# A decayed linear-attention recurrence on TensorE: which operand is stationary, and where the last weights are split

## Chip, core and metric

The kernel runs on one core of a Trainium2 chip. The metric is the time of one execution in device microseconds. Times of stretches are taken from one profiled execution and counted from the start of its span.

## What is computed

Three layers in a row, all in fp32. First a recurrence per batch and head (4 x 8 heads, 768 positions, head dimension 48):

```python
f = 1.0 / (1.0 + np.exp(-f_logit))
for t in range(S):
    state = f[:, :, t, :, None] * state + np.einsum('bhd,bhe->bhde', k[:, :, t], v[:, :, t])
    y[:, :, t] = np.einsum('bhd,bhde->bhe', q[:, :, t], state)
```

Its 3072 rows x of 384 numbers go to a mixture of 8 experts, of which each row takes one:

```python
logits = (x / (norm(x) + 1e-06)) @ (expert_emb / (norm(expert_emb) + 1e-06)).T / tau
expert_idx = np.argmax(logits, axis=1)       # gate_w: its softmax probability
out[mask] = gate_w[mask, None] * (np.maximum(x[mask] @ w1[e], 0.0) @ w2[e])
```

and the result to a bilinear layer: `((x @ w1) * (x @ w2) @ w3) @ w_out`.

## The kernel before, in words

Five engines run programs of their own and meet at semaphores. The recurrence is cut into `NT` = 24 tiles of 128 positions, four batches in turn (`B` = 4), so the state that tile i needs comes from tile i - 4. All 8 heads of a tile are done together, in `NP` = 4 pairs j of two heads g; the two heads of a pair lie in partitions 0 to 47 and 64 to 111. `steps` runs a software pipeline: in step s, TensorE works on scores and products of tile s, cumulative logs of tile s + 2, turning of q and k of tile s + 1 and the output rows of tile s - 1. Each engine has its own `step` with its own order; that order is the queue of the engine.

TensorE's step before, in order: `scores` (stationary kT, 64 rows by 128 columns, moving qT; into two PSUM banks, one for each half of a pair), `cumulate` (running sums of the logs by a triangular matrix), `rows_and_logits` of tile s - 1, `turn_qk` (8 transposes), `state_products`, `update_products` (k times v into `b_s`), `chunk_products`. The output y of a tile is built transposed in the bank `b_y`: the state products have the decayed state (`apart`, 48 columns, the heads of a pair kept apart by zeros) stationary and 128 columns of qT moving; the chunk products have v (48 columns) stationary and the masked scores `am` moving. ScalarE copies this to `yT` (`copy_yT`). `rows_and_logits` makes rows and expert logits of it in one go: yT is stationary, and `pick`, which holds an identity and the expert embeddings, moves with 104 columns. VectorE's `take_rows` copies the rows to `x_ring` and sums the logits; SP stores the rows.

Other names that the steps touch. VectorE: `mask` (scores times the triangle), `bound`, `low_logs`, `copy_kT`, `carry` (new state sum, s_sum), `scale_k` (ks), and `low_w3`. ScalarE: `logs`, `exps`, `copy_qT`, `square` (norms of rows), `high_wo`, `high_w3`. GpSimd: `clamp`, `scale_q` (qs), `decay` (e_half, state and apart from the last row of the decays, which goes by DMA through `last_rows` to `e_all`). SP issues all loads in the order of `stage`; `load_v` waits for the decay of an earlier tile.

Matrices are split in two parts (`_hi`, rounded, and `_lo`, the rest), and `three` multiplies them in three fp32r products. The product w3 @ w_out, `w34_product`, 8 blocks f1 of 24 products, is computed while the routing runs: blocks stand between the steps of the routing in TensorE's order. Its inputs w3 and w_out are loaded and split inside the recurrence's loop: in each step ScalarE makes a half row block high, VectorE the low part. After the recurrence come a flag (whether a decay was too strong, then a slow path), norms (a square root on ScalarE, with a table load), softmax, rank matmuls (L810, L811), lists of rows (L816, L823), gathers by GpSimd, and then the expert slots and the bilinear layer, which the change does not touch.

Of the kernel before, what the change touches and what calls it, by code (L numbers as in the profile page):

```python
# [18 lines left out]
F32 = mybir.dt.float32  # L19
# [17 lines left out]
E = 8  # L37
# [14 lines left out]
TURN_AT = 3  # L52
LISTS = 5
# [11 lines left out]
NORM_AT = 3  # L65
# [9 lines left out]
def steps(eng, step):  # L75

    for s in range(-3, 5):
        step(s, s % 4)
    with eng.Fori(1, NT // 4 - 1) as m:
        for u in range(4):  # L80
            step(m * 4 + (1 + u), (1 + u) % 4, (m, u))
    for s in range(NT - 3, NT + 1):
        step(s, s % 4)
# [24 lines left out]
def build(nc, ctx, qkvf, emb, tau, sets1, sets2, w3_t, w_out, out):  # L108
# [22 lines left out]
    w3_lo = low_w3.enter_context(nc.sbuf_tensor("w3_lo", [P, KF, KF, P], F32R))  # L131
# [7 lines left out]
    def early(name, shape, dt=F32):  # L139
# [3 lines left out]
    early("rest_of_w3_lo", [P, KF * FF - KF * 2 * DM])  # L143
    x_all = early("x_all", [P, (RING + 1) * DM])
    wo_lo = early("wo_lo", [P, KF, DM], F32R)
    above = ExitStack()
    w3_hi = above.enter_context(nc.sbuf_tensor("w3_hi", [P, KF, FF], F32R))
    above.close()
    early("first_w3_hi", [P, FF])
    w3_sb = early("w3_sb", [P, KF, FF])  # L150
# [3 lines left out]
    early("first_wo_hi", [P, DM])  # L154
    wo_sb = early("wo_sb", [P, KF, DM])
    early("up_to_rows", [P, 1216])
# [18 lines left out]
    yT = early("yT", [P, NP * P])  # L175
    state = early("state", [P, B, NP, D])
    apart = early("apart", [P, B, NP, 2, D])
    half = early("half", [P, 2])
    e_half = early("e_half", [P, NP, 2])
# [3 lines left out]
    pick = early("pick", [P, NP, 2 * D + E])  # L183
# [6 lines left out]
    en_sq = early("en_sq", [P, NP, E])  # L190
# [22 lines left out]
    scratch = apart[:].rearrange("p b j g d -> p (b j g d)")  # L213
# [13 lines left out]
    SL = [pick[0:1].rearrange("p j n -> p (j n)")[:, k * (SLOTS + 2) * E:(k + 1) * (SLOTS + 2) * E].rearrange(  # L227
        "p (t e) -> p t e", e=E) for k in range(2)]
# [23 lines left out]
    def mid(name, shape, dt=F32):  # L252
# [17 lines left out]
    bank = [ctx.enter_context(nc.psum_tensor(f"bank{n}", [P, 512], F32)) for n in range(6)]  # L270
    b_cum, b_qT, b_kT, b_y, b_s, b_x = bank
# [16 lines left out]
    w3_hi_done, w3_lo_done = sem("w3_hi_done"), sem("w3_lo_done")  # L288
    masks_done, pads_done = sem("masks_done"), sem("pads_done")
    const_one, const_done, pick_done, emb_turned, en_sq_done, ones_done = (sem(n) for n in (  # L290
        "const_one", "const_done", "pick_done", "emb_turned", "en_sq_done", "ones_done"))
# [5 lines left out]
    sp_done, kv_done, sum_done, half_done, s_done, y_done, yT_done, xl_at = (sem(n) for n in (  # L297
        "sp_done", "kv_done", "sum_done", "half_done", "s_done", "y_done", "yT_done", "xl_at"))
# [1246 lines left out]
```

## Time and profile before

| | |
|---|---|
| median of 3 runs | 728.2 us (727.57 to 729.82) |
| profiled execution | 729.75 us, span 728.0 |
| TensorE busy | 714.8 us, 98% |
| VectorE, ScalarE, GpSimd busy | 350.7, 290.2, 200.3 us |
| granted TensorE clock, mean | 0.997 of full speed |

The page gives the busy time of each engine (PE TensorE, PEld its weight loads, DVE VectorE, ACT ScalarE, POOL GpSimd, SP SyncE), the chain of waits that ended last, and groups of instructions by line. L722 is line 722 of the kernel. The ends of matmuls are modelled, and the durations of neighbours overlap; for a stream of them, the distance from start to start is the cost. The rows below the change are such lines.

### The profile page before, as it was taken

Reading aid. Unit: us, or ns where it says so; the run is one execution under the profiler, and the core shown is the slowest. Engines: PE = TensorE matmul, PEld = TensorE weight load, DVE = VectorE, ACT = ScalarE, POOL = GpSimd, SP = SyncE. Lnnn points to the kernel's source line nnn. Section 1 sums busy time; section 2 is a strip of 40 time slices with the busy share of each in tenths; the row PEclk is TensorE's granted clock in tenths of the full one; section 3 lists DMA queues with packets and bytes.
Section 4 is the critical chain, followed back from the end, with each engine's and each line's share of the span. In section 5 each row is a group of like instructions: output and inputs, shape, how many; then the busy total and the mean of one; then the engine's idle time right before and its main releaser. Section 6 shows DMA issues by size and latency. Waiting matters only on the chain.

```text
span 728.0 us, 14063 instructions
## 1 busy us (share of the span) xinstructions
PE 714.8 (98%) x4911; PEld 655.6 (90%) x4911; DVE 350.7 (48%) x580; ACT 290.2 (40%) x557; POOL 200.3 (28%) x234
## 2 busy tenths in 40 slices
PE   7999999999989999999999999999999999999997
PEld 6999899989989999999999988988988989889887
DVE  6889998768745545455465541211312113112121
ACT  5677788534235534345354442212123022031130
POOL 5756677502320120200000003114033042141242
PEclk9999999999999999999999999999999999999999
DMA  7687886234463454423342440000000000010001
GB/s 220 194 240 212 252 255 158 78 118 122 133 206 96 136 166 131 130 86 109 113 124 86 130 130 1 1 11 33 1 22 22 0 32 11 0 43 0 20 23 43
DMA packets 73057, 70.80 MB, mean 97 GB/s; under 512 B 20520, under 2 KB 61480, under 8 KB 73024
## 3 DMA queue, kind: packets, MB, share of 16 engines
q1 hardware_dynamic: 69952, 60.95, 28.3%
q0 software_dynamic: 3072, 9.44, 4.2%
q8 instruction: 18, 0.29, 0.2%
q14 instruction: 15, 0.12, 0.1%
HBM read 60.88 MB, written 9.49 MB: 97 GB/s over the span
## 4 chain that ended last, share of the span: by engine, by line
PE 82%; DMA 5%; issue 5%; POOL 4%; DVE 2%; SPq 1%; ACT 0%; POOLq 0%; ACTq 0%; DVEq 0%
PE bank L743 14%; PE bank L744 14%; PE bank L745 14%; PE b_a L743 9%; PE b_a L744 9%; PE b_a L745 9%; DMA e_all<-last_rows 4%; PE b_a L673 2%; PE bank L682 2%; PE bank L722 1%; PE bank L702 1%; PE bank L713 1%; POOL apart L554 1%; POOL xs L606 1%; PE bank L834 1%
## 5 line engine op out<-in xcount | busy, mean ns | idle before, releaser
L632 POOL TENSOR_TENSOR p_lo<-prod,p_hi 128x512 fp32r<-128x512 f32 x42 | 53.9, 1283 | 333.3 <-ACT p_hi L1116 333.3
L1113 ACT COPY a_sb<-b_a 128x512 f32<-128x512 f32 x48 | 28.2, 587 | 218.2 <-PE bank L745 218.2
L1494 DVE TENSOR_TENSOR prod<-bank,a_sb 128x512 f32<-128x512 f32 x48 | 33.2, 691 | 165.7 <-ACT a_sb L1113 165.7
L1450 DVE SCALAR_TENSOR_TENSOR h_lo<-b_a,h_hi 128x432 fp32r<-128x432 f32 x64 | 38.8, 607 | 97.2 <-ACT h_hi L1066 97.2
L1066 ACT ACTIVATE h_hi<-b_a 128x432 fp32r<-128x432 f32 x64 | 34.0, 532 | 124.3 <-PE b_a L745 124.0
L1141 DVE TENSOR_TENSOR w_lo<-w_raw,w_hi 128x768 fp32r<-128x768 f32 x72 | 67.9, 956 | 5.3 <-ACT w_hi L1032 1.2
L743 PE MATMUL bank<-h_hi,w_hi 128*128 128x432 f32 x192 | 69.9, 364 | 0.2
L745 PE MATMUL b_a<-x_hi,w_lo 128*128 128x432 f32 x192 | 68.7, 358 | 0.0
L744 PE MATMUL b_a<-x_lo,w_hi 128*128 128x432 f32 x192 | 68.7, 358 | 0.0
L744 PE MATMUL bank<-h_lo,w_hi 128*128 128x432 f32 x192 | 68.7, 358 | 0.0
L745 PE MATMUL bank<-h_hi,w_lo 128*128 128x432 f32 x192 | 68.7, 358 | 0.0
L743 PE MATMUL b_a<-x_hi,w_hi 128*128 128x432 f32 x192 | 68.7, 358 | 0.0
L745 PE MATMUL bank<-w,p_lo 128*128 128x384 f32 x192 | 64.2, 334 | 0.0
L743 PE MATMUL bank<-w,p_hi 128*128 128x384 f32 x192 | 64.2, 334 | 0.0
L744 PE MATMUL bank<-w,p_hi 128*128 128x384 f32 x192 | 64.2, 334 | 0.0
L1032 ACT CAST w_hi<-w_raw 128x768 fp32r<-128x768 f32 x72 | 58.5, 833 | 0.0
L606 POOL DMA_INDIRECT xs<-x_recurrence,ids x24 | 25.9, 1081 | 113.1 <-PE bank L834 80.2
L743 PE MATMUL b_a<-m_hi,w_hi 128*128 128x512 f32 x144 | 56.1, 390 | 0.6 <-DVE w_lo L1141 0.6
L745 PE MATMUL b_a<-m_hi,w_lo 128*128 128x512 f32 x144 | 56.1, 390 | 0.0
L744 PE MATMUL b_a<-m_lo,w_hi 128*128 128x512 f32 x144 | 56.1, 390 | 0.0
L745 PE MATMUL bank<-m_hi,w_lo 128*128 128x512 f32 x144 | 56.0, 389 | 0.0
L744 PE MATMUL bank<-m_lo,w_hi 128*128 128x512 f32 x144 | 56.0, 389 | 0.0
(226 smaller groups left out, 1540.3 us busy)
## 6 DMA issues: line engine op xcount, KB each, us to landing
w_raw<-sets SPq DMA_DIRECT2D x80, 192.0 KB, 3.5
w_raw<-sets SPq DMA_DIRECT2D x40, 384.0 KB, 4.2
ring_all<-qkvf SPq DMA_DIRECT2D x24, 384.0 KB, 4.1
ring_fc<-qkvf SPq DMA_DIRECT2D x24, 192.0 KB, 3.9
ring_all<-qkvf SPq DMA_DIRECT2D x24, 192.0 KB, 3.2
x_recurrence<-x_all SPq DMA_DIRECT2D x24, 192.0 KB, 3.5
w_sb<-w_t SPq DMA_DIRECT2D x8, 512.0 KB, 4.9
wo_sb<-w_out SPq DMA_DIRECT2D x8, 192.0 KB, 4.2
```

Source lines behind the costliest of these rows:

```text
L606: pool.indirect_dma_start(out=xs[:, w % BATCH, :], out_offset=None, in_=rec_dram.rearrange("b c p n -> (b c p) n"), in_offset=bass.Indirec ...
L632: pool.tensor_tensor(p_lo[:, f, :], prod[:, f % 2, :], p_hi[:, f, :].bitcast(F32), ALU.subtract).then_inc(pl_done, 1)
L673: mm = pe.matmul([b_a0, b_a1][g][:, j * P:(j + 1) * P], kT[g * HP:(g + 1) * HP, r % 2, j, :], qT[g * HP:(g + 1) * HP, r % 2, j, :], start= ...
L743: pe.matmul(acc, a_hi, b_hi, start=first, stop=False, skip_group_check=skip)
L744: pe.matmul(acc, a_hi, b_lo, start=False, stop=False, skip_group_check=skip)
L745: return pe.matmul(acc, a_lo, b_hi, start=False, stop=last, skip_group_check=skip)
L1032: act.copy(piece(w_hi, f), piece(w_raw, f)).then_inc(wh_done, 1)
L1066: act.activation(h_hi[:, f % 2, 0:SW], b_h[f % 2][:, 0:SW], ACT.Relu).then_inc(hh_done, 1)
L1113: act.copy(a_sb[:, f % 2, :], b_a[f % 2][:]).then_inc(as_done, 1)
L1141: return dve.tensor_tensor(out_, whole, high.bitcast(F32), ALU.subtract)
L1450: dve.scalar_tensor_tensor(out=h_lo[:, f % 2, 0:SW], in0=b_h[f % 2][:, 0:SW], scalar=0.0, in1=h_hi[:, f % 2, 0:SW].bitcast(F32), op0=ALU.m ...
L1494: dve.tensor_tensor(prod[:, f % 2, :], b_b[f % 2][:], a_sb[:, f % 2, :], ALU.mult).then_inc(pr_done, 1)
```

## The change

- The state products take qT as stationary operand (64 rows by 128 columns) with 48 columns of the undoubled `state` moving; the chunk products take `am` as stationary (128 by 128) with 48 columns of v moving. y comes out in rows, in two banks `b_y0` and `b_y1`. `apart`, `half`, `e_half`, `pick` and `yT` are gone.
- VectorE's `take_rows` copies these rows to `x_ring` straight from the banks. Then `turn_x` transposes them (3 transposes into `b_x`, which `cumulate` uses too), ScalarE copies (`copy_xT_tile`), and a step later `logits` (3 matmuls with the turned rows stationary and 8 columns of embeddings moving) goes into free columns of `b_s`.
- TensorE's order in a step: scores, state products, cumulate, turning of q and k, logits of tile s - 2, turn of the rows of tile s - 1, chunk products, update products. The update of the last four tiles, whose state nobody needs, is left out.
- `scale_k` moves from VectorE to GpSimd (the first tile's stays), which loses two of the three operations of `decay`. `load_v` waits for the update instead of the decay; `load_qk` of a tile is issued one stage later.
- The split of w3 and w_out leaves the loop. w_out is split in two halves in steps 21 to 23 by ScalarE and VectorE (`high_wo`, `low_wo`); w3 in 8 blocks of 1024 columns, high parts by ScalarE from step 21 on and during the routing, low parts by GpSimd, two in the last steps and six ahead of its gathers. Each `w34_product` waits for its own block.
- The flag is found in the last steps, and an extra step NT + 1 holds the last logits.

The core of the diff:

```diff
         def state_products(i, r):
-            need(pe, yT_done, i)
+            need(pe, x_done, i)
             need(pe, s_done, i - B + 1)
             for j in range(NP):
                 for g in range(2):
-                    mm = pe.matmul(b_y[g * HP:g * HP + D, j * P:(j + 1) * P], apart[:, r % 4, j, g, :],
-                                   qT[:, r % 2, j, :], start=(j == 0), stop=False, skip_group_check=True)
+                    mm = pe.matmul([b_y0, b_y1][g][:, j * D:(j + 1) * D], qT[g * HP:(g + 1) * HP, r % 2, j, :],
+                                   state[g * HP:(g + 1) * HP, r % 4, j, :], start=(j == 0), stop=False,
+                                   skip_group_check=True)
             mm.then_inc(sp_done, 1)
...
         def chunk_products(i, r):
             pe.wait_ge(am_done, i + 1)
+            pe.wait_ge(v_landed[r % 4], (i - r % 4) * 4 + 16)
             for j in range(NP):
                 for g in range(2):
                     h = 2 * j + g
-                    mm = pe.matmul(b_y[g * HP:g * HP + D, j * P:(j + 1) * P], ring_v[:, r % 4, h * D:(h + 1) * D],
-                                   am[:, g, j, :], start=False, stop=True, skip_group_check=True)
+                    mm = pe.matmul([b_y0, b_y1][g][:, j * D:(j + 1) * D], am[:, g, j, :],
+                                   ring_v[:, r % 4, h * D:(h + 1) * D], start=False, stop=True, skip_group_check=True)
             mm.then_inc(y_done, 1)
...
-        def rows_and_logits(i):
-
-            pe.wait_ge(yT_done, i + 1)
+        def turned_x(rows):
+            for k in range(KD):
+                mm = pe.transpose(b_x[:, k * P:(k + 1) * P], rows[:, k * P:(k + 1) * P], ident[:])
+            return mm
+
+        def turn_x(i, r):
+
+            pe.wait_ge(x_done, i + 1)
+            pe.wait_ge(bound_done, min(i + 4, NT) if isinstance(i, int) else i + 4)
+            turned_x(x_ring[:, r % 4, :]).then_inc(x_turned, 1)
+
+        def logits_of(acc, xT_rows):
+            for k in range(KD):
+                mm = pe.matmul(acc, xT_rows[:, k * P:(k + 1) * P], en_t[:, k, :], start=(k == 0), stop=(k == KD - 1),
+                               skip_group_check=True)
+            return mm
+
+        def logits(i, r):
+
+            pe.wait_ge(x_copied, i + 1)
+            need(pe, sum_done, min(i + 2, NT - B) if isinstance(i, int) else i + 2)
             need(pe, rl_done, i)
...
+            mm = logits_of(b_s[:, L_AT:L_AT + E], xT_tile[:, r % 2, :])
...
         def step(s, r, part=None):
...
                 scores(i, r)
+                if isinstance(i, int) and i == 0:
+                    pe.wait_ge(pads_done, 2)
+                state_products(i, r)
             if (i := tile_of(s, 2)) is not None:
                 cumulate(i, r + 2)
...
                 turn_qk(i, r + 1)
+            if isinstance(s, int) and s == NT + 1:
+                w34_product(0, range(2, 4))
+            if (i := tile_of(s, -2)) is not None:
+                if isinstance(i, int) and i == 0:
+                    pe.wait_ge(emb_in, 16 * KD)
+                logits(i, r + 2)
+            if isinstance(s, int) and s == NT:
+                w34_product(0, range(2))
+            if (i := tile_of(s, -1)) is not None:
+                turn_x(i, r + 3)
+            if isinstance(s, int) and s == NT:
+                pe.wait_ge(least_done, 1)
+                pe.transpose(b_qT[0:1, 0:P], least_e[:], ident[:]).then_inc(least_turned, 1)
             if (i := tile_of(s, 0)) is not None:
-                if isinstance(i, int) and i == 0:
-                    pe.wait_ge(blank_done, 1)
-                    pe.wait_ge(pads_done, 2)
-                state_products(i, r)
-                update_products(i, r)
                 chunk_products(i, r)
+                if not (isinstance(i, int) and i >= NT - B):
+                    update_products(i, r)
...
+        def scale_k(i, r):
+            if isinstance(i, int) and i == 0:
+                pool.sem_inc(ks_done, 1)
+                return
+            pool.wait_ge(exp_done, i + 1)
+            need(pool, kv_done, min(i - 1, NT - B + 1) if isinstance(i, int) else i - 1)
+            need(pool, tr_done, i - 1)
+            pool.tensor_tensor(ks[:, r % 2, :, 0:D], ring_qk[:, r % 4, DM:2 * DM].rearrange("p (h d) -> p h d", h=H),
+                               en[:, r % 2, :].rearrange("p (h d) -> p h d", h=H), ALU.mult).then_inc(ks_done, 1)
...
+        def low_w3(f1):
+            pool.wait_ge(w3_hi_done, f1 + 1)
+            if f1 >= LOW_HEAD:
+                pool.wait_ge(w3_lo_done, f1)
+            pool.tensor_tensor(w3_lo(f1), w3_raw(f1), w3_hi(f1).bitcast(F32), ALU.subtract).then_inc(w3_lo_done, 1)
...
             if (i := tile_of(s, -1)) is not None:
                 act.wait_ge(x_done, i + 1)
                 need(act, nsq_done, i)
                 square(i, x_ring[:, (r + RING - 1) % RING, :]).then_inc(nsq_done, 1)
-            if part:
-                high_w3(*part)
+            if (i := tile_of(s, 1, 1)) is not None:
+                copy_qT(i, r + 1)
+            if (i := tile_of(s, 2)) is not None:
+                exps(i, r + 2)
+            if (i := tile_of(s, -1)) is not None:
+                copy_xT_tile(i, r + 3)
+            if isinstance(s, int) and s == NT - 3:
+                high_wo(0)
+                high_w3(0)
+            if isinstance(s, int) and s == NT - 2:
+                high_w3(1)
+            if isinstance(s, int) and s == NT - 1:
+                high_wo(1)
+                high_w3(2)
+            if isinstance(s, int) and s == NT:
+                high_w3(3)
```

## Rows read from the trace of the kernel before

**Rows 1.** The page's busy time of TensorE: us, share of the span, instructions.
```profile
PE 714.8 (98%) x4911; PEld 655.6 (90%) x4911; DVE 350.7 (48%) x580; ACT 290.2 (40%) x557; POOL 200.3 (28%) x234
```

**Rows 2.** Busy time by stretches (columns in the first line): first to last scores.
```profile
core 0: us, PE busy (x) PEld busy (x) DVE busy (x) ACT busy (x) POOL busy (x), PEclk, DMA share, GB/s
13.29:144.38 131.09, 130.60 (x1878) 119.60 (x1878) 117.02 (x213) 96.53 (x230) 86.74 (x121) 1.00 0.69 199
```

**Rows 3.** The chain that ended last, one steady step: start us, us, what.
```profile
104.76 1.09 PE b_a L673 x16
105.86 0.38 PE bank L664
106.40 0.87 PE bank L722 x8
107.27 0.87 PE bank L713 x8
108.15 1.01 PE bank L682 x16
109.16 0.45 PE bank L693 x16
109.61 0.88 PE bank L702 x16
```

**Rows 4.** TensorE in order of time: start us, us, instructions; starts of the scores.
```profile
13.29 1.16 PE L673 MATMUL b_a<-qT,kT 64*128 64x128 f32 x16 [0.88 <-DVE kT L1165]
...
35.29 1.16 PE L673 MATMUL b_a<-qT,kT 64*128 64x128 f32 x16
...
41.21 1.16 PE L673 MATMUL b_a<-qT,kT 64*128 64x128 f32 x16
...
87.53 1.16 PE L673 MATMUL b_a<-qT,kT 64*128 64x128 f32 x16 [0.49 <-DVE kT L1165]
...
144.38 1.16 PE L673 MATMUL b_a<-qT,kT 64*128 64x128 f32 x16
```

**Rows 5.** TensorE in order of time, products of the last weights around the rank matmuls.
```profile
156.45 0.33 PE L743 MATMUL b_a<-wo_hi,w_hi 128*128 128x384 f32 x1
...
158.01 0.33 PE L743 MATMUL b_a<-wo_hi,w_hi 128*128 128x384 f32 x1
...
160.11 0.39 PE L810 MATMUL bank<-apart,before 128*128 128x8 f32 x2 [1.42 <-DVE apart L1320]
160.36 0.37 PE L811 MATMUL bank<-apart,ones 128*128 128x8 f32 x2
160.58 0.45 PE L743 MATMUL bank<-wo_hi,w_hi 128*128 128x384 f32 x1
...
163.38 0.53 PE L743 MATMUL bank<-wo_hi,w_hi 128*128 128x384 f32 x1
```

**Rows 6.** Weight loads in order of time, the first of the state products.
```profile
102.35 0.83 PEld L682 LDWEIGHTS bank<-qT,apart 128*48 128x48 f32 x16 [0.17 <-issue]
```

**Rows 7.** VectorE in order of time, at the start.
```profile
5.01 1.22 DVE L1243 COPY pick<-ident 128x384 f32<-128x384 f32 x1
...
6.20 0.51 DVE L1146 TENSOR_TENSOR lg_lo<-lg,lg_hi 128x384 fp32r<-128x384 f32 x1
```

**Rows 8.** GpSimd in order of time, in the steady loop.
```profile
103.50 1.00 POOL L542 TENSOR_TENSOR qs<-ring_all,ec 128x384 f32<-128x384 f32 x1
105.92 0.20 POOL L550 TENSOR_TENSOR e_half<-e_all,half 128x8 f32<-128x8 f32 x1 [1.42 <-DMA e_all<-last_rows]
...
107.34 1.16 POOL L536 TENSOR_SCALAR ring_fc<-ring_fc 128x384 f32<-128x384 f32 x1
```

**Rows 9.** Groups of instructions by line and shape, 0 to 225: busy us, mean ns.
```profile
L1141 DVE TENSOR_TENSOR w_lo<-w_raw,w_hi 128x768 fp32r<-128x768 f32 x16 | 14.9, 953 | 0.8 <-ACT w_hi L1032 0.3
...
L1032 ACT CAST w_hi<-w_raw 128x768 fp32r<-128x768 f32 x16 | 12.6, 834 | 0.0
```

**Rows 10.** ScalarE in order of time, table load and root of the norms.
```profile
154.06 1.28 ACT L1025 ACT_TABLE_LOAD   x1 [1.63 <-DVE flag L1263]
...
155.35 0.23 ACT L1025 ACTIVATE rt<-nsq 128x32 f32<-128x32 f32 x1
```

More of the change, by code:

```diff
@@ L81, in steps @@
             step(m * 4 + (1 + u), (1 + u) % 4, (m, u))
-    for s in range(NT - 3, NT + 1):
+    for s in range(NT - 3, NT + 2):
         step(s, s % 4)
@@ L174, in build @@
     am = early("am", [P, 2, NP, P])
-    yT = early("yT", [P, NP * P])
+    xT_tile = early("xT_tile", [P, 2, DM])
     state = early("state", [P, B, NP, D])
-    apart = early("apart", [P, B, NP, 2, D])
-    half = early("half", [P, 2])
-    e_half = early("e_half", [P, NP, 2])
+    scratch = early("scratch", [P, 8 * NT * E])
     s_sum = early("s_sum", [P, NP, D])
@@ L226, in build @@
         "p (v i) -> p v i", v=3)
-    SL = [pick[0:1].rearrange("p j n -> p (j n)")[:, k * (SLOTS + 2) * E:(k + 1) * (SLOTS + 2) * E].rearrange(
-        "p (t e) -> p t e", e=E) for k in range(2)]
+    SL = [slot_rows[:, k, :].rearrange("p (t e) -> p t e", e=E) for k in range(2)]
     front.close()
@@ L422, in _ @@
         stage(NT // RING - 1, 0)
-        load_v(NT - 3, 1)
-        load_last(NT - 6, 2)
-        save_last(NT - 5, 3)
-        load_qk(NT - 1, 3)
-        for i in range(NT - 4, NT):
-            if i >= NT - 2:
-                load_v(i, i % RING)
+        for i in range(NT - 3, NT):
+            load_v(i, i % RING)
+            load_last(i - 3, (i - 3) % RING)
+            save_last(i - 2, (i - 2) % RING)
+            if i < NT - 1:
+                load_qk(i + 1, (i + 1) % RING)
+        for i in range(NT - 2, NT):
             load_last(i - 1, (i - 1) % RING)
@@ L441, in _ @@
         with sp.If(trips == 1):
-            for k in range(KD):
-                sp.dma_start(en_t[:, k, :], emb[:, k * P:(k + 1) * P].rearrange("e p -> p e"),
-                             allow_slow_non_contiguous=True).then_inc(emb_turned, 16)
             with sp.Fori(0, CH) as c:
@@ L579, in step @@
                 before_clamp(i, r + 3)
[L580 removed]
+            if (i := tile_of(s, -2)) is not None and not (isinstance(i, int) and i >= NT - B):
                 decay(i, r + 2)
@@ L609, in gather @@
                 ).then_inc(gathered, 16)
+        for f1 in range(2, KF):
+            low_w3(f1)
         pool.wait_ge(x_done, NT)
@@ new lines, in take_logits, with low_wo @@
+        def take_logits(i):
+            return dve.tensor_copy(row_of(i), b_x[:, DM:DM + E])
+        def low_wo(half):
+            rows = slice(half * KF // 2, (half + 1) * KF // 2)
+            dve.wait_ge(wo_hi_done, half + 1)
+            low(wo_lo[:, rows, :], wo_sb[:, rows, :], wo_hi[:, rows, :]).then_inc(wo_lo_done, 1)
+        def step(s, r, part=None):
+            if (i := tile_of(s, -1)) is not None:
+                take_rows(i, (r + RING - 1) % RING)
+                if not (isinstance(i, int) and i >= NT - B):
+                    carry(i, r + 3)
+            if isinstance(s, int) and s == NT:
+                for q in range(RING):
+                    dve.wait_ge(last_landed[q], 16 * (NT // RING))
+                dve.tensor_reduce(least_e[:], e_all[:].rearrange("p i j -> p (i j)"), AXX, ALU.min
+                                  ).then_inc(least_done, 1)
```

273 lines of the change are left out of this document (119 added, 154 removed).

## The prediction

> **What bounds the kernel now.** I read the page's busy line first: TensorE is busy over nearly the whole span [rows 1]. A share of that kind is an average, so next came the busy time by stretches: from the first scores to those of the last tile TensorE idles 0.5 us of 131.09, at the full clock, VectorE 14, ScalarE and GpSimd 35 and more [rows 2]. The third view is the chain in the steady loop. It runs down TensorE alone, part after part, and one step of it (one tile of 128 positions) takes from 104.76 to 109.61 + 0.87 = 110.48, so 5.72 us [rows 3]. The starts of the scores confirm it: 13.29 for the first tile, 144.38 for the last, and one stall of 0.49 at 87.53 because the copy of kT came late [rows 4]. So in the recurrence every us of TensorE work added to a step is a us on the end; work taken from the other engines is worth nothing beyond that one stall. After the recurrence TensorE fills the routing with products of the last weights, with one real idle time, 1.42 us before the rank matmuls [rows 5].
>
> **The rate that decides.** An fp32 matmul stands in the trace as two pairs of load and matmul. The 8 instructions of `rows_and_logits` move 104 columns each and take 0.87 us, 0.109 each; the 8 transposes move 128 columns and take 0.87 to 0.88, also 0.109 [rows 3]. With fewer columns the price hardly falls: the extra matmul with `ones` stationary moves 32 columns in two instructions, and its step takes 41.21 - 35.29 = 5.92 instead of 5.72, so 0.10 each [rows 4]; with 8 columns, L810 and L811 take 0.25 and 0.22 for two each, 0.118 on average (the next products are longer, so the second pair may already have met the slower clock) [rows 5]. What these have in common is a stationary operand of 128 rows by 128 columns in fp32. I read it as the load of that operand setting the pace: 0.109 (0.100 to 0.118) per instruction, whatever moves, up to 128 columns. Where two small tiles share the array the price is lower: scores, 64 rows by 128 stationary, 16 in 1.09; state products, 48 stationary columns with 128 moving, 16 in 1.01; chunk products likewise, 0.88; update, 64 stationary columns with 48 moving, 16 in 0.45, 0.028 each [rows 3].
>
> The Trainium skill (TensorE: Matmul & The Clock Gate, LDWEIGHTS) says that a load's time goes by its columns at 1.2 per ns, 107 ns for 128. The trace agrees for the full array, with 0.109. By that figure the sixteen chunk products would be an estimated 1.71 us. The Trainium skill (TensorEngine Tiling (Array Packing), When to Use Tiling) also advises, for a small free dimension, to make the small operand stationary and tile the columns. The kernel before does just that, at 0.88 us, and the change undoes it; by the page alone the change would lose up to a factor of two on these products.
>
> **The change part by part, in one steady step.**
> - Scores: untouched, 1.09. Of it about 0.18 is the pause after products of another tile shape, as before the state products (0.17 idle, issue) [rows 6].
> - State products: still 16 instructions, but the stationary operand is now qT, 64 rows by 128, with 48 state columns moving. Bounds: 0.45 (update row) and 16 x 0.109 = 1.74 (loads of the two halves one after another). The scores have the very same stationary shape and take 1.09 with 128 moving, so the halves do overlap. They follow the scores in the same shape: 1.09 - 0.18 = 0.91, against 1.01 before.
> - Cumulate 0.54, turning of q and k 0.88: the same.
> - `rows_and_logits` goes, -0.87. In its place `turn_x`, 3 transposes: 3 x 0.109 = 0.33, and `logits`, 3 matmuls, 6 instructions with 8 columns: 6 x 0.109 = 0.65. Bounds of the latter 0.17 (6 x 0.028, update row) and 0.71 (6 x 0.118).
> - Chunk products: am becomes stationary, 128 x 128 over the full array, 48 columns move. Bounds 0.45 and 16 x 0.118 = 1.89; 16 x 0.109 = 1.74 by the nearest rows, those of the full array with few columns. Before, 0.88. This is the main term.
> - Update: now behind a full-array group, so it takes the pause: 0.45 + 0.17 = 0.62.
>
> Sum: 1.09 + 0.91 + 0.54 + 0.88 + 0.33 + 0.65 + 1.74 + 0.62 = 6.76 us against 5.72.
>
> The first step lacks turn and logits, the second the logits: 5.78 and 6.11. Steps 2 to 19: 18 x 6.76 = 121.68, and 0.20 for the matmul of the norms. The last four tiles have no update: steps 20 and 21 are 6.14 each, step 22, without cumulate, 5.60. From the first to the last scores this is 151.65 against 131.09: **+20.56**.
>
> **Start.** VectorE's memset of yT and its 1.22 us copy into pick stand ahead of lg_lo; lg_lo started at 6.20, right behind that copy [rows 7]. The chain of waits goes through lg_lo, so what it gains is between 0 and the 1.2 of the copy, less what ScalarE's lg then holds up; I take -0.4. The three emb DMAs that replace eight shorten SP's queue, which nobody waits for here. **Stall at 87.53:** -0.5, since VectorE loses the weight split and scale_k.
>
> **What moves to other engines, at nothing.** VectorE was busy 117.02 us over these 23 steps [rows 2], 5.1 each, and loses more than it gains, of 6.76. Its order holds: take_rows needs the chunk products and has the update and scores (1.7 us) to finish before the state products ask for it. GpSimd loses e_half and apart and gains scale_k: the whole decay before took 107.34 - 105.92 = 1.42, clamp 1.16, qs 1.00, ks about the same, so at most 4.6 us [rows 8]. It works a step ahead: its decay began 1.2 us behind the scores at 104.76, for a turning that comes in the next step. By the order of the new step that turning wants ks 2.5 us in, 9.3 us behind those scores. GpSimd would be through after 5.8; 3.5 us are free. On SP, load_v waits for the update instead of for the decay, which comes earlier; load_qk moves one tile nearer, but is issued more than a step ahead of its use. If the GpSimd cover is gone, each us is a us of the step.
>
> **The tail.** T is the start of the last scores. Before: rank matmuls at 160.11 - 144.38 = T+15.7. Now TensorE works 4.72 to the end of the chunk products. The second half of the w_out split sits in the queues in front of the last rows: ScalarE copies the turned rows of the tile before by T+3.8, then high_wo(1), 1536 elements, twice the 0.83 of 768: T+5.4; VectorE's low_wo(1) waits for it and takes twice 0.95 [rows 9]: T+7.3. Only then take_rows, T+7.9. TensorE, with the logits and six products (0.173 each, nine in 1.56 [rows 5]) done at T+6.4, waits 1.5. Turn, square and copy until T+9.2, high_w3(3) about 1.1, the flag's read about 1 and a table load 1.28: the root at T+12.6, before at T+11.0 [rows 10]. The chain from there to the rank matmuls is unchanged: **+1.6**. Whether the slow clock after the wait (nine products in 2.80 after 160.58 [rows 5]) comes again is open; about 1.5 us less if not. GpSimd's blocks of w3_lo, 1024 elements, some 2.5 us each, stand in front of its gathers. TensorE takes 24 x 0.173 = 4.2 us per block, so they keep ahead; the last ends near T+26.5, the ids come near T+28.5. Slack 2 us, then a us per us.
>
> Total: 20.56 + 1.6 - 0.4 - 0.5 = **+21.3 us**. The profiled execution took 729.75 around its span of 728.0, so its like would be 751.0; the median of the runs is 728.2, and against it the forecast is **749.5**.
>
> **Rivals.**
> - *The load hides, faster.* If a load for full-array products overlapped as in the update row, 0.028 per instruction, chunk and state would be 0.45 each, logits 0.17: a step of 4.53. VectorE and ScalarE then limit at about 5: 24 x (5.0 - 5.72) = -17, time 711. The rest of the step sums to 4.04, so with 25 full-array instructions it turns into a gain once one costs under (5.72 - 4.04) / 25 = 0.067. Nothing above shows it that cheap in fp32; the rows at 8 and 32 columns speak directly against it. 7 in 100 with its milder forms, up to 727.
> - *The two halves of the state products don't overlap.* 1.74 instead of 0.91: 0.83 x 24 = 20 more, 769 to 770. Against it the scores row. 5 in 100.
> - *ks from GpSimd becomes the wait.* It decides if the last-row DMA lands more than 4.7 us behind the scores; it let the decay go at 1.2. With half a us per step, 12 more: 761. 7 in 100.
> - *The change does what it says and the time doesn't show it:* needs the step within 0.1 of 5.72, chance 1 in 100.
>
> **How the numbers follow.** The forecast has 80 in 100. Its own bounds: at 0.100 per instruction, state products 0.85 and no pause before the update, a step is 6.3: 10 less, 739; at 0.118, with the state products at the scores' 1.09, 7.1: 8 more, 758. The range 738 to 760 holds this case nearly whole, and the milder half of a wait on ks. Faster by over 0.3% (about what a measurement of this kernel can tell from no change) has 0.07, within 0.3% 0.02, slower 0.91.
>
> **What would show it.** Chunk products with 16 instructions in 1.6 to 1.9 us; logits near 0.65; state products near 0.9; scores 6.3 to 7.1 us apart; TensorE still without idle time in the loop; and VectorE and ScalarE idler. A step below 5.7 refutes the rate; idle time of TensorE ahead of the ks transposes, the queue reading; a first-to-last distance of 152 with a time outside the range, the tail.

## The result, and the profile of the changed kernel

The changed kernel takes 769.2 us (median of four runs, 767.65 to 769.85), the kernel before 728.0 beside it. The ratio is 1.0558, with an interval from 1.0534 to 1.0582: slower by 41.2 us, where the forecast was slower by 21.3 and the range ended at 760. The profiled execution took 769.85 around a span of 768.0, against 729.75 around 728.0.

The page's busy line and its row of TensorE's granted clock, which answer to [rows 1]:

```profile
PE 748.4 (97%) x4887; PEld 695.3 (91%) x4887; DVE 332.2 (43%) x519; ACT 286.1 (37%) x535; POOL 212.4 (28%) x212
PEclk9999999977899999999999999999999999999999
```

TensorE is as full as before. The clock row says more: three of the 40 slices, from 154 us on, show 7, 7 and 8 tenths. There the recurrence ends and the routing begins.

The chain that ended last, one steady step (start us, us, what), which answers to [rows 3]:

```profile
105.19 1.09 PE b_a L689 x16
106.28 0.83 PE b_y L698 x16
107.10 0.38 PE bank L680
107.48 0.18 PE bank L681
107.66 0.87 PE bank L733 x8
108.53 0.57 PE bank L750 x6
109.10 0.38 PE bank L739 x3
109.48 1.72 PE b_y L721 x16
111.20 0.60 PE bank L711 x16
111.80 1.09 PE b_a L689 x16
```

A step is 111.80 - 105.19 = 6.61 us, before 5.72. Its parts are scores, state products (L698), cumulate, turning of q and k (L733), logits (L750), turning of x (L739), chunk products (L721), update (L711). TensorE alone carries it, as before.

The changed kernel by stretches (each row: us, busy time and instruction count of TensorE, weight loads, VectorE, ScalarE, GpSimd, then the granted clock, DMA share and GB/s), which answers to [rows 2]:

```profile
14.00:152.00 138.00, 137.81 (x1734) 133.38 (x1732) 84.42 (x146) 78.21 (x188) 79.05 (x94) 1.00 0.63 181
...
158.00:160.00 2.00, 0.74 (x14) 0.55 (x10) 0.00 (x0) 1.12 (x2) 0.87 (x2) 1.00 0.44 116
...
162.00:166.00 4.00, 4.00 (x22) 3.91 (x22) 1.52 (x4) 0.61 (x2) 0.00 (x0) 0.50 0.10 36
...
182.00:184.00 2.00, 2.00 (x15) 2.00 (x14) 0.56 (x3) 1.43 (x2) 0.30 (x1) 0.92 0.00 0
```

In the loop TensorE has no idle time worth naming and the full clock; VectorE and ScalarE are at six tenths of it. Then, at 158, TensorE stands still for a while, and from 162 to 182 its clock is at half (0.50, 1.2 GHz). It falls to half twice more, each time behind a wait: for some 6 us behind the one before the rank matmuls, and for some 3 us from 220 on.

The same from TensorE's rows in order of time (start, us, line, operation, what ended the idle time before it): the scores of the last three tiles, the first work after the standstill, and the rank matmuls. They answer to [rows 4, 5]:

```profile
13.54 1.16 PE L689 MATMUL b_a<-qT,kT 64*128 64x128 f32 x16 [0.88 <-DVE kT L1197]
...
151.56 1.16 PE L689 MATMUL b_a<-qT,kT 64*128 64x128 f32 x16
...
157.58 1.16 PE L689 MATMUL b_a<-qT,kT 64*128 64x128 f32 x16
160.99 1.23 PE L698 MATMUL b_y<-state,qT 64*128 64x48 f32 x16 [2.25 <-DVE x_all L1217]
...
169.15 2.08 PE L689 MATMUL b_a<-qT,kT 64*128 64x128 f32 x16
...
192.86 0.59 PE L838 MATMUL bank<-scratch,before 128*128 128x8 f32 x2 [2.47 <-DVE scratch L1358]
```

The scores of tile 21 in the kernel before, the same view:

```profile
133.29 1.16 PE L673 MATMUL b_a<-qT,kT 64*128 64x128 f32 x16
```

So the surplus over the kernel before grows like this. At the scores of tile 21 it is 151.56 - 133.29 = 18.3. At those of tile 23 it is 169.15 - 144.38 = 24.8 [rows 4]. At the rank matmuls it is 192.86 - 160.11 = 32.8 [rows 5], and at the end 768.0 - 728.0 = 40.0. The loop costs about what the forecast said. The other half of the loss arises in its last two steps and behind them, where the forecast had put 1.6.

Two readings of the trace name candidates. The first is the chain of waits ahead of the standstill (start us, us, what); SPq is SyncE's queue:

```profile
156.46 1.16 DMA last_rows<-ec
...
157.64 0.40 SPq L362
...
158.08 2.23 DMA x_recurrence<-x_all
...
160.38 0.57 DVE x_all L1217
```

VectorE's copy of tile 21's rows (L1217) goes into the ring slot of tile 17 and must wait until that is stored. The store stands in SyncE's queue behind all loads of the loop and behind both DMAs of tile 23's last rows, which themselves wait for an exp. So it starts only at 158.08. TensorE needs the bank that the copy empties.

The second is VectorE beside GpSimd during the routing. VectorE, in order of time:

```profile
190.09 2.71 DVE L1358 TENSOR_TENSOR_SCAN scratch<-restart,scratch 128x192 f32<-128x192 f32 x1
...
193.08 1.91 DVE L1363 TENSOR_SCALAR rt<-rt 128x24 f32<-128x24 f32 x1
195.03 0.30 DVE L1364 RECIPROCAL gates<-rt 128x24 f32<-128x24 f32 x1
...
195.57 1.92 DVE L1368 TENSOR_TENSOR_SCAN rt<-ones,rt 128x8 f32<-128x8 f32 x1
...
197.73 2.27 DVE L1370 TENSOR_TENSOR rt<-rt 128x8 f32<-128x8 f32 x1
```

GpSimd, the same time, with the splits of blocks 4 to 7 of the last weights:

```profile
190.03 4.92 POOL L569 TENSOR_TENSOR w_lo_head<-w_all,w_high 128x1024 fp32r<-128x1024 f32 x2 [3.95 <-ACT w_high L1011]
195.10 4.87 POOL L569 TENSOR_TENSOR w_high<-w_all,w_high 128x1024 fp32r<-128x1024 f32 x2
```

In the trace of the kernel before the same four instructions run with GpSimd idle:

```profile
159.50 0.56 DVE L1320 TENSOR_TENSOR_SCAN apart<-restart,apart 128x192 f32<-128x192 f32 x1
...
160.34 0.18 DVE L1325 TENSOR_SCALAR rt<-rt 128x24 f32<-128x24 f32 x1
...
161.09 0.17 DVE L1330 TENSOR_TENSOR_SCAN rt<-ones,rt 128x8 f32<-128x8 f32 x1
...
161.50 0.17 DVE L1332 TENSOR_TENSOR rt<-rt 128x8 f32<-128x8 f32 x1
```

Here they take 2.71, 1.91, 1.92 and 2.27, together 7.7 more. Each of them ends about when an instruction of GpSimd does (the two of the first row at about 192.5 and 195.0, those of the second at about 197.5 and 200.0). The reduce, the reciprocal and the copy out of PSUM (195.36, 0.17) are not stretched.

The rule stands in the Trainium skill (SBUF — State Buffer, SBUF: two separate sides): VectorE and GpSimd share a pair of ports as "an **exclusive lock**, not a bandwidth split", taken on VectorE's side by an instruction in a two-port mode or, against a GpSimd instruction that reads SBUF, by one with two SBUF inputs, and held for a whole instruction. The trace agrees: the four end with GpSimd's instructions, and the reduce and the reciprocal, with one input, and the copy that reads PSUM keep their durations.

### The profile page after: what moved, and what is told of

Its sections match the earlier page's. It is cut to its first block, busy times and chain, and to the rows that moved or that the text cites. A ratio compares the mean times of both kernels' runs of the same rounds, so it can differ in the third digit from the quotient of the medians.

```text
span 768.0 us, 13790 instructions
## 1 busy us (share of the span) xinstructions
PE 748.4 (97%) x4887; PEld 695.3 (91%) x4887; DVE 332.2 (43%) x519; ACT 286.1 (37%) x535; POOL 212.4 (28%) x212
## 4 chain that ended last, share of the span: by engine, by line
PE 87%; issue 4%; DVE 4%; POOL 1%; DMA 1%; ACT 1%; ACTq 0%; DVEq 0%; POOLq 0%; SPq 0%
PE b_a L768 9%; PE b_a L770 9%; PE b_a L769 9%; PE bank L770 8%; PE bank L768 8%; PE bank L769 8%; PE b_y L721 6%; PE b_y L768 5%; PE b_y L770 5%; PE b_y L769 5%; PE b_a L689 3%; PE bank L733 3%; PE b_y L698 3%; PE bank L750 2%; PE bank L711 2%
## 5 line engine op out<-in xcount | busy, mean ns | idle before, releaser
L1488 DVE SCALAR_TENSOR_TENSOR h_lo<-b_a,h_hi 128x432 fp32r<-128x432 f32 x64 | 38.8, 606 | 97.2 <-ACT h_hi L1106 95.8
L768 PE MATMUL bank<-m_hi,w_hi 128*128 128x512 f32 x144 | 56.0, 389 | 0.0
L721 PE MATMUL b_y<-ring_all,am 128*128 128x48 f32 x384 | 48.4, 282 | 0.0
L721 PEld LDWEIGHTS b_y<-ring_all,am 128*128 128x128 f32 x384 | 48.1, 204 | 0.0
L768 PE MATMUL b_y<-h_hi,w_hi 128*128 128x432 f32 x128 | 46.9, 367 | 0.9 <-DVE h_lo L1488 0.6
L770 PE MATMUL b_y<-h_hi,w_lo 128*128 128x432 f32 x128 | 45.8, 358 | 0.0
L769 PE MATMUL b_y<-h_lo,w_hi 128*128 128x432 f32 x128 | 45.8, 358 | 0.0
```

The lines of the kernel that those rows point to most:

```text
L721: mm = pe.matmul([b_y0, b_y1][g][:, j * D:(j + 1) * D], am[:, g, j, :], ring_v[:, r % 4, h * D:(h + 1) * D], start=False, stop=True, skip_ ...
L768: pe.matmul(acc, a_hi, b_hi, start=first, stop=False, skip_group_check=skip)
L769: pe.matmul(acc, a_hi, b_lo, start=False, stop=False, skip_group_check=skip)
L770: return pe.matmul(acc, a_lo, b_hi, start=False, stop=last, skip_group_check=skip)
L1488: dve.scalar_tensor_tensor(out=h_lo[:, f % 2, 0:SW], in0=b_h[f % 2][:, 0:SW], scalar=0.0, in1=h_hi[:, f % 2, 0:SW].bitcast(F32), op0=ALU.m ...
```

## The experiments

Those named a_ start from the changed kernel, those named b_ from the kernel before. Ratios are against the kernel before, run on the same chip, with their interval.

**The load's rate.** Eight more fp32 matmuls a step, with the 128 x 128 identity stationary and 8, 48 or 128 columns moving; they go into a bank that the state products start afresh.

```
+                need(pe, yT_done, i)
+                for _ in range(8):
+                    pe.matmul(b_y[:, 0:8], ident[:], upto[:, 0:8], start=True, stop=True)
```

> The kernel before with 8 more fp32 matmuls per step, stationary 128 by 128, only 8 columns moving. Theory (the load sets the pace): the same 41.9 us more as with 48 columns, span 770. Rival (by moving columns, with a floor): 3 to 11 us more, span 731 to 739.

> The kernel before with 8 more fp32 matmuls in each of its 24 steps, stationary 128 by 128, 48 columns moving, into a bank that is overwritten afterwards. Theory (the load of a 128 by 128 fp32 operand sets the pace at 0.109 per instruction): 16 x 0.109 x 24 = 41.9 us more, span 770. Rival (cost goes by the columns that move, 128 columns in 0.109): 16 x 0.041 x 24 = 15.7 us more, span 744; at the update row's 0.028, 10.8 more.

> The kernel before with 8 more fp32 matmuls per step, stationary 128 by 128, 128 columns moving. Both theories: 16 x 0.109 x 24 = 41.9 us more, span 770, since 128 moving columns take as long as the load. If load and moving were added instead of overlapped: twice as much, span 812.

One run each: 769.5, 768.2 and 770.2 us. The chain shows the sixteen added instructions (L784) in one steady step, with 8 columns and then with 128:

```profile
105.02 1.69 PE bank L784 x16
```

```profile
105.36 1.79 PE bank L784 x16
```

From the first to the last scores the three kernels take 169.4, 170.2 and 171.7 us, against 131.1 before, so 38.3, 39.1 and 40.6 more. Over 23 steps with 16 instructions that is 0.104, 0.106 and 0.110 for each. Sixteen times as many moving columns add 0.006. So for these shapes the columns that move do not set the pace, as the forecast had it, and its 0.109 was slightly too dear for few columns. What the three share is the stationary operand of 128 by 128, whose load the forecast named. Whether it is the load itself, or another cost of every instruction that fills the array, no run separates.

**The orientation of the chunk products alone.**

```
-                    mm = pe.matmul(b_y[g * HP:g * HP + D, j * P:(j + 1) * P], ring_v[:, r % 4, h * D:(h + 1) * D],
-                                   am[:, g, j, :], start=False, stop=True, skip_group_check=True)
+                    mm = pe.matmul(b_y[:, h * HP:h * HP + D], am[:, g, j, :],
+                                   ring_v[:, r % 4, h * D:(h + 1) * D], start=False, stop=True, skip_group_check=True)
```

> The kernel before with one part of the change: the chunk products alone take the masked scores as stationary operand (128 by 128) and move 48 columns of v; they are written in rows into the same bank, so that y, and all that follows, is not the reference's. Theory (0.104 to 0.110 per full-array instruction): 1.66 to 1.76 instead of 0.88 us per step, and up to 0.17 for one more change of tile shape: 24 x (0.8 to 1.05) = 19 to 25 us more, 748 to 753 us. Rival (half the moving columns is a gain): 728 or less.

Measured: 837.3 us, far off. The steady step in the chain of waits, though, shows what was asked:

```profile
103.88 1.92 PE bank L702 x16
```

Sixteen products with 1.92 instead of 0.88: +1.04 a step, of which the pause after products of another tile shape is about 0.2 (1.72 in the changed kernel, where they follow the same shape). Over 23 steps the first and last scores lie 154.5 apart, 23.4 more. The remaining 86 of the 109 us come from the expert stage: with rows that are not y, the routing fills more slots. The page's group of the hidden layer's split, which has x64 and 38.8 us in the kernel before:

```profile
L1450 DVE SCALAR_TENSOR_TENSOR h_lo<-b_a,h_hi 128x432 fp32r<-128x432 f32 x88 | 53.4, 607 | 129.0 <-ACT h_hi L1066 129.0
```

At eight instructions a slot that is 11 slots instead of 8. The run's time says nothing of the change; its step does. That was a fault of the experiment's plan: its expectation took the time downstream as independent of the data.

**The place of the stores.** Each ring slot's store goes up into the last three steps of SyncE's loop.

```
         for i in range(NT - 3, NT):
 ...
             if i < NT - 1:
                 load_qk(i + 1, (i + 1) % RING)
+            store_x((i - RING) // B, (i - RING) % B)
 ...
-        for i in range(NT - 7, NT):
+        for i in range(NT - 4, NT):
```

> The changed kernel with one move on SP's queue: the stores of the rows of tiles 17, 18 and 19 stand right behind the loads of tiles 21, 22 and 23, instead of behind all loads and the last rows' round trips. Theory (the copy of tile 21's rows waited 4.6 us for a ring slot whose store was queued too late, TensorE idled 2.3 us for it, and its clock then stayed at half until 182): the wait goes, 2.3 us and about 10 us of half clock come back, 757 us, spacing of the last scores about 6. Rival (the wait was for the rows' own chain and another wait takes its place, or the clock falls all the same at the light end of the recurrence): 766 to 769 us.

Measured: 757.2 us, ratio 1.0401 (1.0377 to 1.0425). By the ratios that is 11.4 us less than the changed kernel, by the medians 12.0, as expected. TensorE's rows around the former standstill:

```profile
158.24 0.99 PE L699 MATMUL b_y<-state,qT 64*128 64x48 f32 x16
...
162.85 1.16 PE L690 MATMUL b_a<-qT,kT 64*128 64x128 f32 x16
```

No wait, and the full clock up to the last scores (162.85 instead of 169.15). From 168 the clock falls here too (0.50 until 170, 0.68 until 172, then 1.00). The wait of 2.25 us cost 11 to 12 mainly because the steps behind it ran at half clock: the mean granted clock of the four runs is 0.976 to 0.979 in the changed kernel and 0.991 to 0.995 here, and 0.015 of 760 us is an estimated 11 us.

**GpSimd's lock, three ways.** First, its splits in four instructions of 256 columns instead of one of 1024.

```
-            pool.tensor_tensor(w3_lo(f1), w3_raw(f1), w3_hi(f1).bitcast(F32), ALU.subtract).then_inc(w3_lo_done, 1)
+            for q in range(0, KF, 2):
+                ins = pool.tensor_tensor(w3_lo(f1)[:, q:q + 2, :], w3_raw(f1)[:, q:q + 2, :],
+                                         w3_hi(f1)[:, q:q + 2, :].bitcast(F32), ALU.subtract)
+            ins.then_inc(w3_lo_done, 1)
```

> The changed kernel with GpSimd's split of each block of 1024 columns made as four instructions of 256 columns, same place, same work. Theory (an exclusive lock: a VectorE instruction with all operands in SBUF waits until the GpSimd instruction that has begun is over): the four stretched instructions of the rank chain (2.71, 1.91, 1.92, 2.27 us instead of 0.56, 0.18, 0.17, 0.17) lose most of their 7.7 us of waiting, at most 0.6 each is left; 6 to 8 us faster, 761 to 763. Rival (the two engines share a bandwidth): the GpSimd work is the same, so the chain is stretched as much as before, 769 us.

> Both edits. If the steady loop (scores 6.62 to 6.76 us apart against 5.72) is all that the orientation of the products costs, and the rest of the loss stood in these two places: 769 - 12 - 7 = 750 us, the forecast's number. If something else at the end costs as well: 755 us or more. If the two hide each other: about 757.

Measured: 766.6 (1.0534, 1.0512 to 1.0556) alone, 754.8 (1.0385, 1.0358 to 1.0412) together with the stores' new place, so by the medians 2.6 and 2.4 us less, a third of what was expected, and by the ratios only 1.7 and 1.2, with intervals that overlap. Nor did both edits give the 750 that was expected of them. VectorE in order of time, of the kernel with the pieces alone:

```profile
191.60 1.09 DVE L1361 TENSOR_TENSOR_SCAN scratch<-restart,scratch 128x192 f32<-128x192 f32 x1
...
194.68 0.66 DVE L1372 TENSOR_TENSOR rt<-rt 128x8 f32<-128x8 f32 x1
...
196.08 0.85 DVE L1375 TENSOR_TENSOR scratch<-scratch,rt 128x192 f32<-128x192 f32 x1
```

The single waits are short now, but there are many: the two engines take turns, piece against instruction, and what took 0.17 to 0.36 takes 0.66 to 0.85, ten times over.

Second, the splits of blocks 4 to 7 left out altogether (the products take the high parts in place of the low ones), with the stores in their new place.

```
+            if f1 >= 4:
 ...
+                pool.tensor_tensor(w3_lo(f1)[:, 0, 0:8], w3_raw(f1)[:, 0, 0:8], w3_hi(f1)[:, 0, 0:8].bitcast(F32),
+                                   ALU.subtract).then_inc(w3_lo_done, 1)
+                return
```

> The changed kernel with the stores moved as before, and GpSimd's split of w3 blocks 4 to 7 left out (a token of 8 columns stays for the order; the third product of each of these blocks takes the high part instead of the low one, same shape, so the output lacks their low part). Theory (the pieces only gave way to more collisions, twelve of 0.5 us instead of four of 2; what counts is that GpSimd works in SBUF beside the rank chain at all): all stretched instructions of the chain fall back to 0.17 to 0.56, 7.7 us and one idle time of TensorE with its half clock come back, 748 us (747 to 750). Rival (the rank chain does not set the end, TensorE's products do): 755 us or more.

Measured: 748.0 us, 1.0261 (1.0238 to 1.0284), so 10.2 us less by the ratios than with the stores' place alone, 9.2 by the medians. VectorE's chain has its old durations back:

```profile
180.54 0.56 DVE L1365 TENSOR_TENSOR_SCAN scratch<-restart,scratch 128x192 f32<-128x192 f32 x1
...
181.37 0.18 DVE L1370 TENSOR_SCALAR rt<-rt 128x24 f32<-128x24 f32 x1
```

GpSimd's own queue is no rival for this price: with the stores' place alone, its splits end at 189.1, and its first gather, at 198.78, waits for VectorE's ids.

Third, the same splits made later, after the lists of positions are out.

```
-        for f1 in range(2, KF):
+        for f1 in range(2, 4):
+            low_w3(f1)
+        pool.wait_ge(list_in, 1)
+        for f1 in range(4, KF):
             low_w3(f1)
```

> The changed kernel with the stores moved, and GpSimd's blocks 4 to 7 held back until VectorE has made the list of the rank chain, nothing left out. Theory: the chain is free, but the fifth product waits about 1.8 us for its block, the gathers start some 7 us later and VectorE's later instructions collide instead: between the two, 750 to 754 us. Rival: the held blocks and late gathers cost more than the chain gains, 757 us or more.

Measured: 756.6, 1.0381 (1.0359 to 1.0404): almost nothing against 1.0401, and above the 750 to 754 that was expected. The chain up to the rank matmuls is free of the lock. The held splits then meet VectorE's later instructions, of which one (L1407) takes 2.76 us, and the gathers of GpSimd stand behind them. Of this kernel, VectorE's row with the ids, and then a row of GpSimd's splits and its first gather:

```profile
192.74 0.60 DVE L1404 CAST ids<-rt 128x4 int32<-128x4 f32 x1
```

```profile
193.46 5.29 POOL L570 TENSOR_TENSOR w_high<-w_all,w_high 128x1024 fp32r<-128x1024 f32 x2
198.92 1.20 POOL L620 DMA_INDIRECT xs<-x_recurrence,ids  x1 [0.17 <-issue]
```

The ids are ready at 193.3, the gather starts at 198.9, right behind the splits. So here the same work costs mostly by its place in GpSimd's own queue. Neither the smaller pieces nor the later place brought back most of the 9 to 10 us. That work which ends before the root of the norms, or is done on another engine, would be free is a guess; no run shows it.

**The half clock by itself.** Even with both causes gone, the clock fell once more. The kernel with the splits left out, by stretches:

```profile
166.00:168.00 2.00, 2.00 (x19) 2.00 (x18) 0.29 (x1) 2.00 (x3) 0.00 (x0) 0.91 0.04 9
168.00:170.00 2.00, 2.00 (x8) 2.00 (x8) 2.00 (x3) 0.65 (x2) 1.30 (x1) 0.50 0.00 0
```

No idle time stands before it: TensorE shows 2.00 busy of 2.00. What it did there was the work of the last steps: scores and transposes (128 columns moving), state and chunk products (48) and logits (8), without the two matmuls of 384 columns that cumulate the logs in every step of the loop. The clock was back at 1.00 from 178 on. Two kernels test whether it also falls with wide matmuls among these: four matmuls of 384 columns, whose results nobody reads, in each of the last three steps with logits.

```
+            if isinstance(s, int) and NT - 2 <= s <= NT:
+                pe.wait_ge(x_copied, s - 1)
+                for _ in range(4):
+                    pe.matmul(b_x[:, 0:DM], upto_r[:], lg_hi[:, 0, :], start=True, stop=True)
```

> The kernel of a_clean (its low parts left out as there) with 4 more fp32r matmuls of 384 moving columns in each of steps 22, 23 and 24, into a bank that is overwritten: 12 x 0.173 = 2.1 us of added work. In a_clean the granted clock fell to half at 167.8 without any idle time of TensorE, while the last steps had lost their cumulates and moved 8 to 48 columns per instruction; it stayed there for 10 us. Theory (it falls for want of moving columns, not for idleness): the fall doesn't come or is shorter, 748 + 2.1 - 5 = 745 us. Rival (the fall has another cause): 750 us and the same half clock.

> The changed kernel with the same 12 matmuls and nothing else. There the clock was at half from 161 to 182, from the wait for the stores to the first products of the last weights. Theory (wide matmuls bring it back): it rises within steps 22 or 23, some 3 to 8 us come back, 763 to 768 us. Rival (narrow or wide makes no difference, only time without idleness does): 12 x 0.32 = 3.8 us more, 773 us.

Added to the kernel without the splits, they gave 749.8 us (1.0291, 1.0265 to 1.0318); added to the changed kernel as it is, 772.1 (1.0613, 1.0583 to 1.0644). A stretch of the first and then two of the second:

```profile
168.00:170.00 2.00, 2.00 (x18) 2.00 (x17) 0.74 (x1) 2.00 (x2) 0.00 (x0) 1.00 0.01 4
```

```profile
180.00:184.00 4.00, 4.00 (x16) 3.96 (x15) 0.84 (x4) 0.62 (x2) 2.26 (x1) 0.50 0.13 49
184.00:188.00 4.00, 4.00 (x22) 3.85 (x21) 0.80 (x5) 2.67 (x3) 1.56 (x1) 0.73 0.00 0
```

In the first the clock stays full all the way, and the mean granted clock is 1.000 in all four of its runs, against 0.993 to 0.999 without the wide matmuls (on another chip). So with wide matmuls among the others the fall did not come. The time did not get shorter, though: the intervals overlap, and the 745 that was expected was missed.

That does not make the full clock worthless. Without the wide matmuls, the four runs of one and the same kernel show it: mean clocks of 0.993, 0.995, 0.997 and 0.999 go with 750.3, 748.0, 748.1 and 745.8 us, so 0.006 of 748 us, an estimated 4.5 us of TensorE's work, comes back as 4.5 us. The 10 us at half clock belong to the slowest of the four, which was the profiled one; the length of the fall differs from one execution to the next. Against the run at 0.999, the wide matmuls cost some 4 us. Of these, 12 x 0.17 = 2.0 are their own work and 1.3 more idle time (by the rows of stretches from 170 to 230, TensorE idles 2.6 us there and 1.3 without them); the rest I could not place.

In the second kernel the clock, once at half behind the standstill, does not come back from four wide matmuls a step, and the time is 3 to 4 us longer, as its rival expectation had it (3.8). The clock rises only among the products of the last weights, which are all of that width, as in the changed kernel. What exactly it takes to raise it stays open.

**A better version of the kernel before.** The standstill ahead of its rank matmuls and the half clock behind it [rows 5] can be covered: products of the last weights are pulled in front of the wait for the flag, and the updates of tiles 21 to 23, whose state nobody reads, are left out with their carry and decay.

```
-                update_products(i, r)
+                if not (isinstance(i, int) and i >= NT - B):
+                    update_products(i, r)
 ...
+        w34_product(2, range(3))
 ...
-        w34_product(2)
+        w34_product(2, range(3, KF))
```

> The kernel before, orientation untouched, with two small parts: the update, carry and decay of the last tiles (21 to 23), which nobody needs, left out (3 x 0.45 = 1.35 us of TensorE), and the first nine products of the third block of last weights put ahead of the wait for the rank matmuls, into TensorE's idle 1.42 us. Theory (TensorE's work and its one idle time set the end, and the half clock after 160.58 came from that idle time): -1.35 - 1.4 - 1.4 = -4.2, 724 us, and no half clock in the routing. Rival (the rank chain, not TensorE's work, sets the routing's end): -1.35 or less, 727.

Measured: 726.3 us, ratio 0.9975 (0.996 to 0.9989), 2 us better than the kernel before. Of this kernel, the stretch where the clock had been lowest:

```profile
160.00:164.00 4.00, 4.00 (x25) 4.00 (x24) 3.79 (x10) 0.48 (x1) 0.00 (x0) 1.00 1.01 274
```

In the kernel before the clock of this stretch is 0.61. Less was gained than the 4.2 us expected, and 726.3 lies nearer the rival's 727 than 724. TensorE's waits there fell from 1.4 and 2.1 us (rank matmuls, gathered rows) to 0.3 and 2.1, by the view of waits of both, so 1.1 and not 1.4 came back from them; the rest of the difference was not traced.

## Why the forecast was half right

**The rate and the step: right.** The forecast had 0.109 us for every instruction with a full fp32 stationary operand, and 6.76 for a step. Part by part, forecast against the steady step shown above: scores 1.09 and 1.09, state products 0.91 and 0.83, cumulate 0.54 and 0.56, turning of q and k 0.88 and 0.87, logits 0.65 and 0.57, turning of x 0.33 and 0.38, chunk products 1.74 and 1.72, update 0.62 and 0.60. The halves of the state products overlap even better than in the scores, since 48 columns move and not 128. The logits go with the rate for 8 columns, 6 x 0.096. The kernels with eight more matmuls confirm the rate apart from this change. The chunk products are the main term, as said.

**The loop: 18.5 instead of 20.56.** From the first to the last scores the kernel with neither the standstill nor the late splits takes 162.65 - 13.05 = 149.6. The 18 steady steps took 6.65 on average (144.41 - 24.77 over 18), 2.0 us in total below the forecast. One misreading stands against that: "The last four tiles have no update" is true of three only, the step of tile 20 still has its update and took 6.61 instead of 6.14. GpSimd's ks never became a wait, and the stall at 87.53 is gone, as said. But the forecast counted that stall twice: the 131.09 of before contains it, the 151.65 does not, and -0.5 was subtracted once more. The step of the upper bound sums to 7.17 and not 7.1, which puts the bound at 759, still inside the range. The start gained nothing that can be told from the spread: first scores at 13.54 in the changed kernel and between 11.70 and 13.55 in its variants; before it is 13.29, and between 11.75 and 13.35 in the variants of that kernel.

**The tail: +1.6 forecast, about 22 measured.** Here two steps failed.
- The queue of SyncE. For `take_rows` the forecast asked only for its source ("needs the chunk products") and for the time until the state products ask for it; on SyncE's queue it followed what `load_v` and `load_qk` wait for, and not the stores behind them. The ring slot's wait stood in the sum at nothing. The stores had been in that order before as well, and there no copy of rows waited for one. What changed is who waits: y's rows are copied into the ring of stored rows straight from the bank that TensorE needs next, so the slot's store is now in front of TensorE. Price: 11.4 us by the ratios, of it 2.25 of standstill; most of the rest is the half clock behind it, which the forecast knew from [rows 5] but had weighed at 1.5.
- "The chain from there to the rank matmuls is unchanged", and the splits on GpSimd "keep ahead". The forecast compared GpSimd's durations with the times at which TensorE needs the blocks, and these were right: 2.35 to 2.99 for a block, forecast 2.5. It did not ask what GpSimd's work does to VectorE beside it. Before, GpSimd had nothing to do beside the routing, so no row of before showed it. Price: 10.2 us by the ratios. Where the lock stayed out of the chain up to the rank matmuls (the splits made later), these start 180.21 - 163.21 = 17.0 behind the last scores, against 15.7 before: the +1.6 itself was well sized, at 1.3. In the changed kernel they start 23.7 behind. GpSimd's first gather in the kernel before, with its idle time:

```profile
172.73 1.21 POOL L606 DMA_INDIRECT xs<-x_recurrence,ids  x1 [27.22 <-DVE ids L1362]
```

**The sum.** By the ratios, of 40.6 us 11.4 are the stores' place and 10.2 the splits beside the routing. The 19.0 that are left (1.0261) are the order of the operands in the loop and a small tail. Each of the two prices is a difference of ratios that are known to about 0.24% each, so to some 2.5 us. In spans the kernel with both causes gone is 748.4 - 728.0 = 20.4 longer, of which 162.65 - 144.38 = 18.3 had been lost at the last scores; the tail is then 2.1, and the forecast's 1.6 would have been fair for it. Its predicted time, 749.5, is within 2 us of that kernel, in part by luck: the loop was 2.0 too dear, the tail, the start and the stall together too cheap. The direction and the mechanism of the loop were right, and what failed was the claim that nothing else in the tail becomes late.

**The rivals.** *The load hides* is refuted by the rows at 8, 48 and 128 columns, *the halves don't overlap* by 0.83; that its 769 to 770 is the measured time is chance, and the time alone would have spoken for it. *ks* did not wait. None of them had the tail; the range, bounded at 760 by the rate's errors, was built on the term that was sure and not on the one that was unsure.

## What to carry to other kernels

With fp32 operands, count instructions with a full stationary operand, not moving columns: with 8 to 128 columns each cost 0.104 to 0.110 us here, so the small operand belongs on the stationary side, where two tiles share the array.

When a result goes into another buffer, follow that buffer's release as far as its last user's queue, in the last steps of the loop above all, where loads no longer alternate with stores.

Before moving work to GpSimd, list VectorE's instructions that will run beside it. Where they formed a chain of small ones, the move cost 10.2 us for splits that take 9.8, and cutting each of these in four gave back 1.2 to 2.6. Holding them back instead put them in front of GpSimd's own gathers.

## What the hardware showed unexpectedly

- TensorE's clock fell to half without any idle time in the rows before it (at about 167.8, TensorE 2.00 of 2.00 busy), in the last steps of the recurrence, whose matmuls move 8 to 128 columns. With twelve matmuls of 384 columns among them it stayed at 1.00. The same twelve did not raise it once it was at half.
- A lock between VectorE and GpSimd that shows in no list of waits: the instruction is recorded as busy for 2.71 us instead of 0.56. One finds it only by comparing durations of the same form.
- One kernel's executions differ by how long the clock stays low: 0.993 to 0.999 on average, 750.3 to 745.8 us. A single profile can show the longest fall, as it did here.
